# Two fp32 feed-forward layers behind a seven-tap mix: identity products in TensorE's start pauses, weight remainders taken at other times, ScalarE's exp and table load placed earlier

## What is computed

```python
# attention-like mix: softmax over 7 taps, then a causal weighted sum of rows of x
w = exp(weight_gen - max(weight_gen)); w = w / (sum(w) + 1e-9)
out[s, head] = sum_k w[s, head, k] * x[s - 6 + k, head]        # 2 x 4096 tokens, 192 channels, 8 heads
# layer 1, gated, d_ff 1536
xn = out / sqrt(mean(out * out) + 1e-6) * rms_g
y = (silu(xn @ w_gate) * (xn @ w_val)) @ w_out
# layer 2, d_ff 2048
h = y @ w_in
result = (h * sigmoid(1.702 * h)) @ w_out2
```

## Time and profile before

| | us |
|---|---|
| median of 3 runs | 1231.42 (1231.39 to 1232.36) |
| the profiled execution | 1231.47 |
| its span, first to last instruction | 1229.5 |
| mean granted clock of TensorE | 0.999 of full speed |

### The profile page before, as it was taken

One profiled execution on the slowest core, in us unless ns is written; L12 is line 12 of the kernel. 1 busy time (PEld: TensorE's weight loads), 2 busy tenths in 40 slices (PEclk: granted clock), 3 DMA queues, 4 the chain that ended last, 5 costly groups with the idle time before them and its releaser, 6 DMA issues.

```text
span 1229.5 us, 28927 instructions
## 1 busy us (share of the span) xinstructions
PE 1218.8 (99%) x12013; PEld 1128.1 (92%) x12013; DVE 773.4 (63%) x1203; ACT 682.0 (55%) x1222; POOL 60.0 (5%) x65
## 2 busy tenths in 40 slices
PE   8999999999999999999999999999999999999998
PEld 5889999999998999999889999998999999899998
DVE  8886474855748566484764848557485674944533
ACT  5656555465554655546565464655545556464554
POOL 4613000000000000000000000000000000000000
PEclk9999999999999999999999999999999999999999
DMA  7311010100101000010010100000010000000000
GB/s 206 105 45 34 18 33 2 47 4 18 33 5 46 2 18 34 11 40 2 18 33 18 33 2 27 24 18 33 5 48 1 18 33 2 14 1 15 1 15 14
DMA packets 15457, 33.09 MB, mean 27 GB/s; under 512 B 1893, under 2 KB 8805, under 8 KB 15329
## 3 DMA queue, kind: packets, MB, share of 16 engines
q1 hardware_dynamic: 15328, 31.26, 7.8%
HBM read 24.96 MB, written 6.29 MB: 25 GB/s over the span
## 4 chain that ended last, share of the span: by engine, by line
PE 93%; DVE 3%; issue 2%; ACT 1%; POOL 0%; DMA 0%; DVEq 0%; ACTq 0%; POOLq 0%
PE up_ps L976 45%; PE acc L976 34%; PE acc L980 7%; PE up_ps L980 6%; DVE hidden L926 1%; POOL out_w L493 0%; ACT h_hi L658 0%; DVE h_lo L935 0%; PE acc L1241 0%; ACT hidden L651 0%; DVE mixed_eps L751 0%; ACT silu L635 0%; DMA logits<-in_weight_gen_dram 0%; POOL rms_stat L501 0%; DVE mixed_eps L779 0%
## 5 line engine op out<-in xcount | busy, mean ns | idle before, releaser
L935 DVE TENSOR_TENSOR h_lo<-hidden,h_hi 128x512 fp32r<-128x512 f32 x448 | 314.0, 701 | 357.6 <-ACT h_hi L658 356.2
L658 ACT CAST h_hi<-hidden 128x512 fp32r<-128x512 f32 x448 | 278.1, 621 | 244.6 <-DVE hidden L926 232.2
L976 PE MATMUL acc<-out_w,h_hi 64*128 64x384 f32 x1024 | 301.9, 355 | 0.7 <-DVE y_f L873 0.7
L980 PE MATMUL acc<-out_w,h_hi 64*128 64x384 f32 x1024 | 301.8, 355 | 0.0
L651 ACT ACTIVATE hidden<-up_ps 128x512 f32<-128x512 f32 x256 | 152.8, 597 | 190.3 <-PE up_ps L980 190.0
L976 PE MATMUL acc<-out_w,h_lo 64*128 64x192 f32 x1024 | 253.1, 247 | 0.0
L980 PE MATMUL acc<-out_w,h_lo 64*128 64x192 f32 x1024 | 253.0, 247 | 0.0
L976 PE MATMUL up_ps<-x_hi,up_w 64*128 64x512 f32 x752 | 236.7, 394 | 0.0
L980 PE MATMUL up_ps<-x_hi,up_w 64*128 64x512 f32 x752 | 234.8, 392 | 0.0
L976 PE MATMUL acc<-h_hi,out_w 64*128 64x512 f32 x576 | 195.7, 393 | 1.6 <-POOL up_w L493 1.0
L980 PE MATMUL acc<-h_hi,out_w 64*128 64x512 f32 x576 | 195.2, 392 | 0.0
(11 more groups left out here) (145 smaller groups left out, 3190.9 us busy)
## 6 DMA issues: line engine op xcount, KB each, us to landing
x_win<-in_x_dram SPq DMA_DIRECT2D x14, 960.0 KB
out_dram<-out_sb SPq DMA_DIRECT2D x15, 384.0 KB, 4.4
stage<-in_moe_w_out_dram SPq DMA_DIRECT2D x13, 192.0 KB, 2.7
logits<-in_weight_gen_dram SPq DMA_DIRECT2D x16, 112.0 KB, 2.0
stage<-in_moe_w_in_dram SPq DMA_DIRECT2D x4, 256.0 KB, 3.3
stage<-in_moe_w_gate_dram SPq DMA_DIRECT2D x3, 256.0 KB, 3.9
stage<-in_moe_w_gate_dram SPq DMA_DIRECT2D x5, 128.0 KB, 4.0
stage<-in_moe_w_val_dram SPq DMA_DIRECT2D x5, 128.0 KB, 3.9
```

The source lines that it names most:

```text
L658: nc.scalar.copy(h_hi[:, u % 4, :], hidden[:, u % 2, :]).then_inc(hi_ready, 1)
L935: nc.vector.tensor_tensor(h_lo[:, u % 4, :], hidden[:, u % 2, :], h_hi[:, u % 4, :].bitcast(F32), ALU.subtract).then_inc(lo_ready, 1)
L976: return nc.tensor.matmul(ps, w[TOP], data[TOP], start=start, stop=stop)
L980: return nc.tensor.matmul(ps, w[LOW], data[LOW], start=start, stop=stop)
```

## The change

Four edits. TensorE issues six more identity products between the second and the third `leave`, and three more behind `turn_x(0)`. ScalarE does the exp of group 1 (`mix_exp(1)`) ahead of `round_main(0)` and the table load for silu right behind it, and rounds chunk 7 before the first unit; the hi parts of later chunks are rounded behind other units (`HI_BEHIND`, `HI_BLOCK1`). GpSimd makes the remainder of chunk 5 only when y_rest is done, makes 16 and 17 behind the mix of group 1, and makes 18 to 31 ahead of `rms(2)` without waiting for the mix of group 2; 32 and 33 keep their place. VectorE's `mul1` of group 1 moves from ahead of the first unit into unit 0's slot, and `add2` from slot 2 to slot 3.

```diff
-    AHEAD = ["mul0", "mul1"]
-    MIX_SLOT_0 = {0: ["mul2"], 1: ["add1"], 2: ["mul3", "add2"], 3: ["mul4"], 4: ["add3", "mul5"],
+    AHEAD = ["mul0"]
+    MIX_SLOT_0 = {0: ["mul1", "mul2"], 1: ["add1"], 2: ["mul3"], 3: ["add2", "mul4"], 4: ["add3", "mul5"],
...
-    HI_FIRST = 7
-    HI_BEHIND = (9, 11, 13, 15, 17, 19, 21, 21, 22, 23, 24, 26)
+    HI_FIRST = 8
+    HI_BEHIND = (10, 12, 14, 15, 17, 18, 20, 20, 21, 22, 23, 24)
+    HI_BLOCK1 = {2: (24, 25), 3: (26, 27), 4: (28,), 5: (29,), 6: (30,), 7: (31,), 9: (32,), 10: (33,)}
     HELD = CHUNKS1 + SLOTS
-    HI_LATE = 3
...
             rms(0)
             pool.wait_ge(mix, mix_count(0, "scale"))
-            for n in range(LEFT[-1] + 1, CHUNKS1):
+            split_chunk(LEFT[-1] + 1)
+            pool.wait_ge(x_ready, 2)
+            for n in range(LEFT[-1] + 2, CHUNKS1 - 2):
                 if has_lo(n):
                     split_chunk(n)
             rms(1)
             pool.wait_ge(mix, mix_count(1, "scale"))
-            for n in range(CHUNKS1, CHUNKS1 + SLOTS // 2):
+            for n in range(CHUNKS1 - 2, CHUNKS1):
                 split_chunk(n)
-
             pool.wait_ge(x_ready, 4)
-            for n in range(CHUNKS1 + SLOTS // 2, HELD):
+            for n in range(CHUNKS1, len(chunks) - 2):
                 split_chunk(n)
             rms(2)
             pool.wait_ge(mix, mix_count(2, "scale"))
-            for n in range(HELD, len(chunks)):
+            for n in range(len(chunks) - 2, len(chunks)):
                 split_chunk(n)
...
+            mix_exp(1)
             act.wait_ge(g_ready, 2)
             round_main(0)
+            nc.scalar.activation(warm[:, :], g_main[:, :], ACT.Silu)
             copy_left(2)
             copy_twin(0)
-            mix_exp(1)
-            nc.scalar.activation(warm[:, :], g_main[:, :], ACT.Silu)
-            chunk_hi_half(HI_POOL + 1)
+            for n in range(HI_POOL + 1, HI_FIRST):
+                chunk_hi_half(n)
...
-            for a in range(len(LEFT)):
-                leave(a)
+            leave(0)
+            leave(1)
+            rehearse(up_ps[3], 6)
+            leave(2)
             turn_x(0)
+            rehearse(up_ps[3], 3)
```

More of the change, by code:

```diff
@@ L661, in run @@
                             chunk_hi_half(n)
-                    if i == 1 and HI_LATE <= u < HI_LATE + len(chunks) - HELD:
-                        chunk_hi_half(HELD + u - HI_LATE)
+                    for n in HI_BLOCK1.get(u, ()) if i == 1 else ():
+                        chunk_hi_half(n)
                     if mixing and i and u == SQUARE:
```

## The result

The changed kernel takes **1233.59 us**, the median of 22 runs (1233.34 to 1234.68); the kernel before took 1231.73 us beside it (22 runs, 1231.39 to 1232.7). The ratio is 1.0014, 95% interval 1.0008 to 1.0021. So the change costs 1.86 us, clear of zero by its interval. That lies inside the 0.2% (2.5 us) that the prediction took for no change, on the slower side, and inside its range of 1228.0 to 1237.8. The profiled execution took 1233.55 us, its span is 1231.7 us, 2.2 us more than before.

The account below looks back on a forecast made before the run. TensorE, busy 1218.8 of 1229.5 us, was taken to bound the kernel. From 1231.47 us, -0.5 + 3.0 + 1.4 - 0.4 = +3.5 us gave 1235.0 us; the forecast's own range was 1232.5 to 1238, the overall range 1228.0 to 1237.8.

Parts of the forecast that it names:

- Identity products: Start of the kernel: six products take 1.3 us and three 0.65 us, fitting TensorE's 1.4 and 0.8 us pauses; cost 0.
- the fast value: Identity products at the start: 0.22 us each instead of 0.46 us, taken because the full clock is granted there.
- The clock: TensorE from 21.12 to 24.58 us: staying at the full clock gains 1.6 us at that point.
- The sum by the Trainium skill's advice: Keeping TensorE fed so the clock stays up: sum 1.6 us smaller, forecast 1233.4 us.
- VectorE's chain: Block 0 to unit 0: `h_lo` ends at about 28.3 us as before, the clock's gain becomes waiting; gain 0.
- The rest of block 0: Moving chunks 16 and 17 brings group 1's `scale` 1.0 us earlier; block 1's mix starts 0.5 us earlier: -0.5 us.
- Block 1's mix: Eight remainders make VectorE wait 6.6 us up to unit 19's `h_lo`; TensorE loses +3.0 us, bounds +0.7 and +4.3.
- `scale`: Group 2's `scale`, with 0.4 us of room, comes about 5 us late before TensorE's transposes: +1.4 us, bounds 0 and 2.5.
- Behind the mix: From 102 to 112 us two of eight remainders stay; the 0.7 us wait behind y_f shrinks: -0.4 us.
- faster: Rival, chance 0.20: block 1's 2.7 us of room takes the remainders, only the start counts: 1228.2 us.
- No change: Rival, chance 0.23: lower bounds for block 1's mix and `scale`, middle for block 0: -0.2 us, 1231.3 us.
- VectorE always first: Shared port: VectorE goes first whenever both engines want it; the block 1 and `scale` losses fall away: 1230.6 us.

Follow-up runs that it names:

- e3: The kernel before with only the nine identity products added: 1231.54 us, -0.10 us against the kernel before.
- e2: The changed kernel without its nine identity products: 1234.23 us, +2.59 us against the kernel before.
- e5: The kernel before with only the remainders of chunks 16 and 17 moved behind the mix of group 1: 1232.24 us, +0.45 us against the kernel before.
- e4: The kernel before with only GpSimd's remainders of chunks 26 to 31 made early, without waiting for group 2's mix: 1233.76 us, +2.12 us.
- e1: The changed kernel with the remainders of chunks 26 to 33 back behind the mix of group 2: 1230.42 us; run again, 1230.61 us.
- e10: e1 with VectorE's order of block 0 as in the kernel before (`mul1` ahead of the first unit, `add2` in slot 2): 1231.10 us.
- e11: e1 without GpSimd's wait for y_rest ahead of chunk 5: 1230.54 us.
- e12: e1 without the nine identity products: 1230.80 us.
- e6: The changed kernel with GpSimd waiting for `h_lo` of unit 0 before chunk 6: 1233.52 us, +1.73 us against the kernel before.
- e7: The changed kernel with remainders 26 and 27 behind `add6` of group 2 and 28 to 31 behind its reciprocal root: 1234.29 us.

## Why the prediction was right, and where it was not

The forecast was +3.5 us and the median moved by 1.86, on the side forecast; by the prediction's own bound of 2.5 us the result lies within no change, which had a chance of 0.27 against 0.55 for slower. The mechanism is the one forecast, the size about half. By the profiled executions: block 0 -1.09 where -0.5 stood, block 1 +3.81 where 3.0 + 1.4 stood, behind it -0.65 where -0.4 stood, and 0.13 at the first pair. All three terms missed to the same side.

1. *Identity products.* Right: the six take 1.33 us (15.37 to 16.70), they fit, and the first pair is 0.13 us late. Cost 0 within what a trace tells. The reason given for the fast value does not hold, as the ten at the start took 0.46 us each at a granted clock of 1.00 too (1.5 to 6 us); why they are slower stays open.
2. *The clock.* Right as to its place: 1.00 from 21 to 24.6 us. The 1.6 us that it gives there shrink to 0.1 us (e3) and 0.64 us (e2). The sum by the Trainium skill's advice to keep TensorE fed ("TensorE: Matmul & The Clock Gate", "Why this matters for your kernels") had kept them in full.
3. *VectorE's chain.* Right in its main claim: the clock's gain turned mostly into a wait at the first down product, 1.61 us. The size, a gain of 0, was off. Measured from the first pair, `h_lo` of unit 0 ends 0.5 us earlier than before (28.01 - 19.29 against 28.36 - 19.16), and by e2 the clock is worth 0.6 us in the changed kernel and by e3 0.1 to 0.2 without the other moves. The step asked only whether VectorE would be late in any case. It didn't ask what VectorE does once `mul1` stands behind `hidden`: then the chain begins with TensorE's first unit, and the clock counts.
4. *The rest of block 0.* The sign was right; one term was wrong and one gain came for another reason. `scale` of group 1 ends 1.14 us earlier (53.64 - 19.29 against 54.65 - 19.16) where 1.0 stood, and e5 gets 1.08 with 16 and 17 alone. The 0.5 us by which chunks 18 to 23 were to hold VectorE around y_f did not come: they start at 61.91, and TensorE takes 17.39 us from the transposes on where it took 17.34. That turns -0.5 into some -1.1. The 1.0 us wait went too, but e5 keeps it: 16 and 17 stood at 41.78, behind it. The list of waits puts it down to GpSimd; the remainder at 38.05 ended at 39.34, though, and the product at 39.98 started 0.10 us behind the end of `h_lo`. That remainder had waited 0.75 us for ScalarE's rounding and so came to lie in front of `h_lo`. In the changed kernel GpSimd makes it together with the one before:

```profile
34.01 3.00 POOL L493 TENSOR_TENSOR up_w<-stage,up_w 128x512 fp32r<-128x512 f32 x2
```

The runs with ScalarE's old order (e3, e4, e5) start it at 38.0 to 38.3 us and have the wait; e1, e10, e11 and e12, with the new order, start it earlier and do not. The other moves are excluded one by one (VectorE's order e10, chunk 5 e11, the products e12, 16 and 17 e5). So ScalarE's earlier rounding is the likely cause; it was not tried by itself.
5. *Block 1's mix.* Right, and shown by e1 and e4. Forecast were 6.6 us of shut-out; the seven steps add up to 5.4. TensorE came 2.2 us late to the transposes where 3.0 stood, so the room was 3.2 us, as counted (2.7 + 0.65), and the mis-sized term is the shut-out. I had let each remainder hold VectorE for nearly its whole length; the rows show an excess of 0.2 to 1.1 us for one, because part of it lies beside `hidden`. TensorE's stops for `h_lo` and `hidden` came as foretold, but only from 87.7 us on and too short for the list of waits.
6. *`scale`.* Right: a wait of 1.61 us where 1.4 stood. In the forecast it was a small addition to step 5; in the rows it is what sets all 3.8 us, since `scale` is 4.2 us late and had 0.4 us of room.
7. *Behind the mix.* The 0.7 us wait at 113 us is gone and the rest of the span is 0.65 us shorter, a little more than the 0.4 forecast. With 26 to 33 back in their place (e1) there is none of this gain.

The rival "faster" needed less than 3.3 us of waiting in block 1; there TensorE pays 3.8. The room that it counted on was there for `h_lo`, but not for `scale`, which had 0.4 us, so only 1.4 to 1.6 us of shut-out were absorbed. "No change" took the lower bounds of steps 5 and 6 and fell with the same number. The rule of the Trainium skill ("SBUF — State Buffer", "Who interferes with whom") by which GpSimd's instruction holds VectorE out for its whole length is what block 1 shows: the stretched steps end 0.8 us behind the end of a remainder, where the prediction had read 0.54 us for the shorter `h_lo`. Its counterpart, VectorE always first, would have given 1230.6 us and is excluded by e4.

## What to carry to other kernels

Work on GpSimd that shuts VectorE out costs what VectorE has no room for, wherever it stands: count, for each place, VectorE's own work up to its next deadline (here `scale`, not `h_lo`) and put only as many remainders there as the room takes (two were free, eight cost 3.8 us). A wait that goes away where two engines share a bound comes back a few units later (e6), so read the distance between two fixed instructions and not the list of waits. And a higher clock, or an earlier step, gains only where the engine next in the chain is waiting for it: of the 1.6 us that the nine products save on the spot, the stretch of block 0 kept 0.2 us in the old order (e3) and 0.6 us in the new one (e2).

## What was not expected

**The clock falls in some executions only.** Over its 99 runs beside the experiments the kernel before had a mean granted clock of 1.000 in 22, 0.999 in 42, 0.998 in 2, 0.997 in 27 and 0.996 in 6, with medians of 1231.64, 1231.64, 1232.11, 1232.15 and 1232.52 us. The changed kernel had 1.000 in 15 and 0.999 in 7 of its 22 runs; e2, without the products, had 1.000 in 3 (1233.76), 0.999 in 6 (1234.32) and 0.998 in 2 (1235.4). e12, also without them, had 1.000 in 3 of 11, and e1 again, with them, in 8 of 11. So with the same program and the same short pauses the lower level comes or stays away, and the products make it rarer. In the kernel before and in e2 a lower mean goes with a longer time; in the changed kernel it doesn't (median 1233.66 us at 1.000, 1233.40 at 0.999).

**Which pauses it followed.** In e7 TensorE paused 3.1 us at the transposes and the clock was 0.83 over the ten microseconds around it; the changed kernel paused 1.61 us in the same place and kept 1.00. e10, with 1.59 and 0.62 us close together in block 0, did not keep it, and e12 paused 0.8 us at the first pair and 1.61 us at the first down product and did. The ten microseconds from 100 us, e7 and then the changed kernel:

```profile
100.00:110.00 10.00, 6.89 (x56) 5.38 (x54) 6.80 (x9) 4.47 (x8) 4.92 (x5) 0.83 0.01 2
```

```profile
100.00:110.00 10.00, 8.39 (x80) 6.19 (x78) 6.36 (x11) 6.14 (x12) 3.35 (x3) 1.00 0.01 2
```

With it goes a loss behind the transposes: in e7 the rest of the span took 1127.7 us, 1.5 more than in the changed kernel. The granted clock was 0.57 from 104.9 to 107 us and 0.60 to 109, by which I estimate 1.7 us (2.1 x 0.43 + 2.0 x 0.40), so the clock can be all of it; it was not separated.

**Casts are held too.** VectorE's CAST of y_hi has one input, and took 1.52 us beside a remainder (e7); the cast of 64x512 took 1.23, 1.24 and 1.41 us (e7, e5) where it takes 0.41 alone in the changed kernel. I had reckoned with instructions of two inputs, and with casts only at the start of block 0.
